# The first layer of the last experts as block products over pairs of blocks, with the token loop outermost

## The reference

```
N, D, E, F = 3072, 384, 4, 1024
p = domain_probs / (domain_probs.sum(-1, keepdims=True) + 1e-09)
for e in range(E):
    h = np.maximum(x @ w1[e], 0.0)          # first layer, 384 -> 1024
    out += p[:, e:e + 1] * (h @ w2[e])      # second layer, 1024 -> 384
```

## Time and profile before

| | |
|---|---|
| median of 3 runs | 1463.51 us (1460.65 to 1465.16) |
| the profiled execution's own time | 1463.24 us |
| its span, first to last instruction | 1461.3 us |
| mean granted clock of TensorE over the span | 0.997 |
| TensorE busy | 1430.0 us, 98% |
| VectorE, ScalarE, GpSimd busy | 609.7, 501.2, 584.0 us |

### The profile page before, as it was taken

How to read it: one execution, slowest core, us unless ns; L and a number is a source line. 1 busy time by engine, 2 the same in 40 slices (tenths; PEclk the granted TensorE clock), 3 DMA queues, 4 the chain that set the end, 5 groups by cost and what they waited for, 6 DMA issues and landing times.

```text
span 1461.3 us, 25799 instructions
## 1 busy us (share of the span) xinstructions
PE 1430.0 (98%) x10296; PEld 1319.9 (90%) x10296; DVE 609.7 (42%) x933; ACT 501.2 (34%) x975; POOL 584.0 (40%) x552
## 2 busy tenths in 40 slices
PE   4899999999999999999999999999999999999999
PEld 4889999999999999998999999999999999999998
DVE  7585556565565555113333333333333333333332
ACT  6564545454545544213222222222222222222220
POOL 6385545454454544344324323234133143232220
PEclk9999999999999999999999999999999999999999
DMA  8312222212131221110000010010010000100011
GB/s 309 116 53 104 85 72 76 81 54 102 53 102 54 85 72 33 44 44 0 1 32 13 0 44 0 0 44 0 0 43 0 23 20 0 43 0 0 22 43 65
DMA packets 31109, 70.65 MB, mean 48 GB/s; under 512 B 5168, under 2 KB 14128, under 8 KB 31024
## 3 DMA queue, kind: packets, MB, share of 16 engines
q1 hardware_dynamic: 31024, 69.43, 13.9%
HBM read 64.70 MB, written 4.72 MB: 48 GB/s over the span
## 4 chain that ended last, share of the span: by engine, by line
PE 94%; DVE 2%; ACT 2%; issue 1%; DMA 1%; SPq 0%; DVEq 0%; ACTq 0%
PE PS L671 28%; PE PS L661 27%; PE PS L617 21%; PE PS L627 10%; PE PS L565 4%; PE PS L588 2%; PE PS L584 1%; PE PS L568 1%; DMA raw<-in_w_gate 1%; ACT QX L771 1%; PE PS L573 1%; DVE KQ L883 0%; PE PS L596 0%; PE PS L601 0%; ACT AT L748 0%
## 5 line engine op out<-in xcount | busy, mean ns | idle before, releaser
L1147 POOL TENSOR_TENSOR XS_0l<-x2T,XS_0h 128x1536 fp32r<-128x1536 f32 x24 | 84.5, 3521 | 263.5 <-ACT XS_0h L816 263.5
L1037 DVE SCALAR_TENSOR_TENSOR acc<-PS,prob,acc 128x384 f32<-128x384 f32 x192 | 118.7, 618 | 162.0 <-PE PS L671 162.0
L1147 POOL TENSOR_TENSOR XS_1l<-x2T,XS_1h 128x1536 fp32r<-128x1536 f32 x23 | 80.8, 3515 | 252.5 <-ACT XS_1h L816 252.5
L771 ACT ACTIVATE QX<-KQ 48x256 f32<-48x256 f32 x288 | 120.7, 419 | 130.2 <-DVE KQ L883 107.4
L857 ACT ACTIVATE H_1h<-PS 128x512 fp32r<-128x512 f32 x96 | 57.4, 598 | 311.7 <-PE PS L661 311.7
L857 ACT ACTIVATE H_0h<-PS 128x512 fp32r<-128x512 f32 x96 | 57.3, 599 | 299.5 <-PE PS L661 299.3
L1045 DVE SCALAR_TENSOR_TENSOR H_1l<-PS,H_1h 128x512 fp32r<-128x512 f32 x96 | 66.4, 692 | 196.9 <-ACT H_1h L857 196.9
L1045 DVE SCALAR_TENSOR_TENSOR H_0l<-PS,H_0h 128x512 fp32r<-128x512 f32 x96 | 66.1, 692 | 188.7 <-ACT H_0h L857 188.7
L883 DVE TENSOR_TENSOR KQ<-KQ,TOT 112x512 f32<-112x512 f32 (+1 forms) x126 | 110.7, 902 | 46.0 <-PE PS L565 27.9
L976 DVE TENSOR_TENSOR hid<-PS,hid 128x384 f32<-128x384 f32 x96 | 53.5, 557 | 149.2 <-PE PS L617 133.8
L565 PE MATMUL PS<-QX,KQ 112*64 112x64 f32 x1920 | 82.1, 237 | 23.9 <-ACT QX L771 23.1
(11 more groups left out here) (157 smaller groups left out, 4105.0 us busy)
## 6 DMA issues: line engine op xcount, KB each, us to landing
row<-in_rows SPq DMA_DIRECT2D x24, 768.0 KB, 4.4
KQ<-in_qk SPq DMA_DIRECT2D x24, 448.0 KB, 4.1
V<-in_v SPq DMA_DIRECT2D x24, 384.0 KB, 4.8
rawA<-in_w SPq DMA_DIRECT2D x8, 768.0 KB, 4.6
rawB<-in_w SPq DMA_DIRECT2D x8, 768.0 KB, 6.3
A<-in_alpha SPq DMA_DIRECT2D x24, 224.0 KB, 2.7
out_y<-acc SPq DMA_DIRECT2D x5, 768.0 KB, 3.5
raw<-in_w_gate SPq DMA_DIRECT2D x3, 768.0 KB, 12.2
```

What stands on the lines that cost most here:

```text
L771: done = nc.scalar.activation(QX[p][rows, :, g, :].rearrange("d a (n t) -> d a n t", t=2 << level), right, ACT.Copy)
L1037: dve.scalar_tensor_tensor(out=acc[:, n, :], in0=PS[:, result_banks[u], 0:DM], scalar=weight, in1=acc[:, n, :], op0=ALU.mult, op1=ALU.add) ...
L1147: nc.gpsimd.tensor_tensor(XS[c % 2][1][:], x2T[:, :, at:at + T2], XS[c % 2][0][:].bitcast(F32), ALU.subtract).then_inc(xsl_ready, 1)
```

## The change

The unit of work becomes 1024 tokens (two halves of 512) by 256 hidden values (two blocks of 128) of one expert. The groups of 1024 tokens (`q`, three) are the outermost loop; inside are the four experts and their four units each, 48 units in all, so all weights are loaded three times.

Over two of the three blocks of `x` the first layer of a unit is the product of a 2 x 2 matrix of weight blocks and a 2 x 2 matrix of token blocks. It is computed by a scheme with seven block products instead of eight, from sums and differences of blocks: `T1_` to `T4` of `x`, `S1` to `S4` of the weights. The third block (`X31`, `X32`, `W13`, `W23`) is multiplied in the usual way and summed into the same banks. `PRODUCTS` lists the pairs of each of eight groups. The four results are sums of these groups: VectorE adds banks up in a buffer `mixed` in SBUF (`combine`), after ScalarE has copied the first product there. ScalarE rectifies a finished part twice, once into the high part `H2..h` and once in place; GpSimd subtracts (`low_h`). GpSimd also forms the sums of weights and tokens (`w_mix`, `x_mix`) and all low parts, ScalarE all high parts.

TensorE alternates one group of `first` with one block of `second` of the unit before, now eight blocks of six matmuls each; VectorE adds each block to `acc`, which now holds 1024 tokens, twice. The pieces of the next 1024 tokens (nine blocks, four of them sums) are prepared in the first units of a group after the schedule `LATER` (for each unit: blocks to split, sums to form). Those of the first group and the first weights are prepared beside the last dense tile. Stores of a finished group of tokens go out during the next one.

The diff, cut to its core (buffers, semaphores and loop ends are left out):

```diff
-FH = 512
-FCH = FH // P
+FP = 2
+UNITS = F2 // (FP * P)
 T2 = 512
-SUB = T2 // P
-TILES2 = N // T2
-PASSES = E * (F2 // FH)
+PAIR_T = 2 * T2
+SUB = PAIR_T // P
+GROUPS2 = N // PAIR_T
+ALL_UNITS = GROUPS2 * E * UNITS
...
+X11, X21, X31, T3, X22, X32, T1_, T2_, T4 = range(9)
+W11, S3, W12, W22, W13, W23, S1, S2, S4 = range(9)
+X_ORDER = (X11, X21, X31, T1_, X22, X32, T3, T2_, T4)
+T_ORDER = (T1_, T3, T2_, T4)
+PRODUCTS = (
+    ((W11, X11),),
+    ((S2, T2_),),
+    ((S3, T3),),
+    ((S1, T1_),),
+    ((W12, X21), (W13, X31)),
+    ((W22, T4), (W23, X31)),
+    ((S4, X22), (W13, X32)),
+    ((W23, X32),),
+)
+P1, P6, P7, P5, R11, R21, R12, R22 = range(8)
+COMBINED = 8
+PARTS = ((0, 0), (1, 0), (0, 1), (1, 1))
+SUMS = {P6: ((1, 0),), P7: ((2, 1),), P5: ((1, 1), (3, 2)), R11: ((0, 0),), R21: ((2, 2),), R12: ((1, 1),), R22: ((3, 3),)}
+SELF = {P7: 1, P5: 2, R12: 3, R22: 4}
...
+LATER = (((X11, X21), (T1_,)), ((X31, T1_), ()), ((X22,), (T3,)), ((X32, T3), (T2_,)), ((T2_,), ()), ((), (T4,)), ((T4,), ()), ((), ()))
...
-            def first(e, c, j, f):
-
-                wait_count(pe, rl_ready, nth(e, c, j, FCH, f + 1 - FCH))
-                for n in range(KD):
+            def first(q, e, u, g):
+
+                if g < R11:
+                    wait_count(pe, combined, nth(q, e, u, COMBINED, R11 + g + 1 - COMBINED))
+                elif g == R11:
+                    pe.wait_ge(p1_kept, nth(q, e, u, 1, 1))
+                else:
+                    pe.wait_ge(combined, nth(q, e, u, COMBINED, {R21: 1, R12: 2, R22: 4}[g]))
+                terms = [(w, x, c) for w, x in PRODUCTS[g] for c in SPLITS]
+                for at, (w, x, (cw, cx)) in enumerate(terms):
+                    mm = pe.matmul(PS[:, hidden_banks[g % 4], :], W1[u % 2][cw][:, w, :], XB[q % 2][cx][:, x, :],
+                                   start=at == 0, stop=at == len(terms) - 1)
+                mm.then_inc(first_done, 1)
...
+            def second(q, e, u, at):
+
+                wait_count(pe, acc_ready, nth(q, e, u, SUB, at + 1 - 4))
...
-                        mm = pe.matmul(PS[:, hidden_banks[f], :], W1[c // TILES2][w][:, n, f * P:(f + 1) * P],
-                                       XS[c % 2][x][:, n, :],
-                                       start=(n == 0 and (w, x) == SPLITS[0]), stop=(n == KD - 1 and (w, x) == SPLITS[-1]))
-                mm.then_inc(first_done, 1)
-
-            def second(e, c, j, u):
-
-                wait_count(pe, acc_ready, nth(e, c, j, SUB, u + 1 - SUB))
-                for f in range(FCH):
-                    for w, x in SPLITS:
-                        mm = pe.matmul(PS[:, result_banks[u], 0:DM], H2[c % 2][x][:, f, u * P:(u + 1) * P],
-                                       W2[c // TILES2 % 2][w][:, f, :],
-                                       start=(f == 0 and (w, x) == SPLITS[0]), stop=(f == FCH - 1 and (w, x) == SPLITS[-1]))
+                        mm = pe.matmul(PS[:, result_banks[at % 4], 0:DM], H2[u % 2][x][:, f, at * P:(at + 1) * P], W2[u % 2][w][:, f, :],
+                                       start=(f == 0 and (w, x) == SPLITS[0]), stop=(f == FP - 1 and (w, x) == SPLITS[-1]))
                 mm.then_inc(second_done, 1)
 
...
-                for f in pieces:
-                    first(e, c, j, f)
+            def unit(q, e, u, groups=range(len(PRODUCTS)), alone=False):
+
+                if 0 in groups:
+                    pe.wait_ge(w1_ready, nth(q, e, u, 1, 1))
+                    if u == 0 and (not isinstance(e, int) or e == 0):
+                        pe.wait_ge(xb_ready, 9 * (q + 1))
+                for g in groups:
+                    first(q, e, u, g)
                     if alone:
                         continue
-                    if f == 0:
-                        if (c - 1) % TILES2 == 0:
-                            pe.wait_ge(w2_ready, e * 2 + ((c - 1) // TILES2 + 1))
-                        pe.wait_ge(rl_ready, nth(e, c, j, FCH, 0))
-                    second(e, c - 1, j, f)
...
-            tile(B - 1, 1, attend=False, follow=False, ahead=lambda: tile2(0, 0, alone=True, pieces=range(2)))
+                    if g == 0:
+                        pe.wait_ge(w2_ready, nth(q, e, u, 1, 0))
+                        pe.wait_ge(rl_ready, nth(q, e, u, len(PARTS), 2 - len(PARTS)))
+                    if g == SUB // 2:
+                        pe.wait_ge(rl_ready, nth(q, e, u, len(PARTS), 0))
+                    second(q, e, u - 1, g)
...
+            tile(B - 1, 1, attend=False, follow=False, ahead=lambda: unit(0, 0, 0, groups=(P1, P6), alone=True))
...
-            expert(0, alone=True)
-            with pe.Fori(1, E) as e:
-                expert(e)
-            pe.wait_ge(rl_ready, PASSES * TILES2 * FCH)
-            for u in range(SUB):
-                second(E - 1, 2 * TILES2 - 1, 0, u)
+            unit(0, 0, 0, groups=range(P7, R22 + 1), alone=True)
+            pe.wait_ge(x2_ready, TILES1)
+            for u in range(1, UNITS):
+                unit(0, 0, u)
+            for q in range(GROUPS2):
+                with pe.Fori(int(q == 0), E) as e:
+                    for u in range(UNITS):
+                        unit(q, e, u)
+            pe.wait_ge(w2_ready, ALL_UNITS)
...
+            def high_w1(q, e, u):
+
+                if not (isinstance(e, int) and (q, e, u) == (0, 0, 1)):
+                    wait_count(act, first_done, nth(q, e, u, len(PRODUCTS), -len(PRODUCTS)))
+                act.wait_ge(s_ready, nth(q, e, u, 4, 4))
+                nc.scalar.activation(W1[u % 2][0][:, 0:6], rawA[u % 2][:], ACT.Copy)
+                nc.scalar.activation(W1[u % 2][0][:, 6:9], w_sum[:], ACT.Copy).then_inc(w1_high, 1)
+
+            def high_w2(q, e, u):
+
+                wait_count(act, second_done, nth(q, e, u, SUB, -SUB))
+                act.wait_ge(rawB_in[u % 2], nth(q, e, u, 1, 0) * 8 + (16 if u % 2 == 0 else 8))
+                nc.scalar.activation(W2[u % 2][0][:], rawB[u % 2][:], ACT.Copy).then_inc(w2_high, 1)
...
+            def unit(q, e, u, blocks=(), last=False):
+
+                wait_count(act, rl_ready, nth(q, e, u, len(PARTS), 1 - len(PARTS)))
+                act.wait_ge(first_done, nth(q, e, u, len(PRODUCTS), P1 + 1))
+                nc.scalar.activation(mixed[:, 0, :], PS[:, hidden_banks[0], :], ACT.Copy).then_inc(p1_kept, 1)
+                if not last:
+                    high_w1(q, e, u + 1)
+                high_w2(q, e, u)
+                for block in blocks:
+                    high_x(q + 1, block)
+                for at, (m, n) in enumerate(PARTS):
+                    act.wait_ge(combined, nth(q, e, u, COMBINED, R11 + at + 1))
+                    nc.scalar.activation(H2[u % 2][0][:, m, n * T2:(n + 1) * T2], mixed[:, part_of(m, n), :], ACT.Relu)
+                    nc.scalar.activation(mixed[:, part_of(m, n), :], mixed[:, part_of(m, n), :], ACT.Relu).then_inc(rh_ready, 1)
...
-            def add_result(e, c, u, e_of_c):
-
...
-                dve.scalar_tensor_tensor(out=acc[:, n, :], in0=PS[:, result_banks[u], 0:DM], scalar=weight,
-                                         in1=acc[:, n, :], op0=ALU.mult, op1=ALU.add).then_inc(acc_ready, 1)
-
...
+            def combine(q, e, u, g):
+
+                if g == P1:
+                    return
+                done = nth(q, e, u, COMBINED, 0)
+                bank = PS[:, hidden_banks[g % 4], :]
+                if g == P6:
+                    dve.wait_ge(p1_kept, nth(q, e, u, 1, 1))
+                    wait_count(dve, rl_ready, nth(q, e, u, len(PARTS), -1))
+                if g == P5:
+                    wait_count(dve, rl_ready, nth(q, e, u, len(PARTS), 0))
+                if g in SELF:
+                    dve.wait_ge(combined, done + SELF[g])
+                dve.wait_ge(first_done, nth(q, e, u, len(PRODUCTS), g + 1))
+                for to, x in SUMS[g]:
+                    dve.tensor_tensor(mixed[:, to, :], bank, mixed[:, x, :], ALU.add).then_inc(combined, 1)
...
+            def add_result(q, e, u, at, fresh=False):
+
+                dve.wait_ge(second_done, nth(q, e, u, SUB, at + 1))
...
+                else:
+                    dve.scalar_tensor_tensor(out=to, in0=result, scalar=weight, in1=to, op0=ALU.mult, op1=ALU.add).then_inc(acc_ready, 1)
...
+            def unit(q, e, u):
+                for g in range(len(PRODUCTS)):
+                    combine(q, e, u, g)
...
+                        add_result(q, e, u - 1, g, fresh)
...
-            def low_x(e, c):
-
-                pool.wait_ge(const_in, 16)
-                pool.wait_ge(xsh_ready, nth(e, c, 0, 1, 1))
...
-                nc.gpsimd.tensor_tensor(XS[c % 2][1][:], x2T[:, :, at:at + T2], XS[c % 2][0][:].bitcast(F32),
-                                        ALU.subtract).then_inc(xsl_ready, 1)
...
+            def x_low(q, block):
+
+                pool.wait_ge(xb_high, 9 * q + X_ORDER.index(block) + 1)
+                high, low = (t[:, block, :] for t in XB[q % 2])
```

(77 more changed lines are left out.)

257 lines of the change are left out of this document (127 added, 130 removed).

## The result

| | before | changed |
|---|---|---|
| median | 1463.28 us (1460.65 to 1465.16, 4 runs) | **1438.3 us** (1436.23 to 1439.41, 4 runs) |
| ratio | | 0.9829, 95% interval 0.981 to 0.9848 |
| profiled execution: time, span | 1463.24, 1461.3 | 1438.04, 1436.2 |

The forecast was 1439 (1438.8 for the profiled execution), its range 1428 to 1453. In a second set, on another chip, the changed kernel took 1437.67 us, ratio 0.983 (0.9817 to 0.9844).

What follows compares the result with a forecast made beforehand. TensorE, busy for 98% of the span, was taken to bound the kernel. From 1463.24 us, -33.4 + 0.8 + 0.3 + 6.5 + 1.4 = -24.4 gave 1438.8, as a median 1439 us, range 1428 to 1453.

Steps and rivals of the forecast that it cites:

- The matmuls: Expert stage on TensorE: 144 first-layer matmuls go at 0.232 us each, -33.4 us, leaving a unit of 16.07 us.
- The start: First unit of the stage: GpSimd has no head start, so TensorE waits from 661.6 for low part h1, +6.5 us.
- the end is the same chain: End of the kernel: last block, addition of 0.62 us and DMA of 192 KB as before, at no cost.
- P1: Start of the stage: TensorE waits for R11's bank until ScalarE has kept the first product, +0.3 us.
- The clock: After the idle at the start TensorE resumes at the 1.2 GHz level: +1.4 us, at most 2.8.
- Units with three token pieces: Three such units inside the stage: pieces ahead on GpSimd's queue make h1 late by up to 0.3 us, +0.8 in all.
- A: Rival: matmul groups on TensorE cost something at each change, +0.24 us a unit, +12, so 1451 us; chance 0.12.
- B: Rival: GpSimd is 10 to 15% slower than its profile rows, delaying h1 and the start: 1448 us; chance 0.10.
- C: Rival: GpSimd's queue becomes the bound from a stretch of 1.29; 128-wide L1076 showed 1.71; about 1700 us; chance 0.11.
- D: Rival: small waits of half a microsecond in each unit give the saving back: within 0.3% of 1463; chance 0.03.
- So the loss isn't repeated: After the start's wait, GpSimd ends h1 of unit 1 at 683.6 and TensorE wants it from 684: no second wait.
- The work beside the last dense tile: First token splits and weights are hidden beside the last dense tile at no cost; +4 us should this cover fail.

Runs made afterwards that it cites:

- Experiment 1: Changed kernel with P1's three matmuls issued twice in every unit, so 36 first-layer matmuls as before the change: 1470.41 us, ratio 1.0055 to the kernel before.
- experiment 9: Changed kernel with weights and P1 of unit 0 made before the dense layer ends, and token pieces spread over units 2 to 10: 1429.02 us, ratio 0.9776.
- Experiment 6: Changed kernel with three more unused 768-column GpSimd subtractions in each unit: 1581.18 us, ratio 1.0817 to the kernel before.
- experiment 7: Changed kernel with two unused 512-wide VectorE additions, both operands in SBUF, in each unit: 1444.15 us, ratio 0.9873 to the kernel before.
- experiments 2 to 4: Changed kernel, cumulatively: first unit's low parts of H before token pieces, 1437.19 us; first unit's weights split earlier, 1434.86; P1 kept before x2T's copy, 1435.03.
- experiments 8 and 9: Changed kernel with token pieces at most two a unit, units 2 to 10: 1433.8 us; also unit 0's weights and P1 made earlier: 1429.02 us.

## Why the prediction was right

**The matmuls.** Forecast: -33.4, a unit of 16.07. From the stage's 780.5 us take the two waits (6.2 and 0.4) and the low clock (1.7, below): 772.2 for 48 units, 16.09 each. 805.6 - 772.2 = 33.4. Experiment 1 puts the saving back and finds the tile of before to 0.01 us (16.77 in all three token groups, so the three matmuls are worth 0.70 us in two of them and 0.67 in the other). This is the whole of the gain.

**The start.** Forecast: the second low part of H at 668.1, TensorE idle from 661.6 for 6.5 us. Measured: 667.27, and a hole of 6.2. The steps stand in the chain with nearly constant distance: low parts of the first weights done 659.34 (660.1 forecast), second weights 661.15 (661.9), pieces 664.82 (665.6). All are 0.8 early, 0.64 of it because the stage began at 650.60 instead of 651.24, an offset of the execution (in experiment 9 the stage began at 651.36); what follows the last matmul took 0.6 longer (3.5 for 2.9 us of the span), so that the two cancel. The second is no offset: every profile of a changed kernel has it, and "the end is the same chain" put it at nothing. Its cause wasn't looked for.

**P1.** Forecast +0.3, measured 0.4.

**The clock.** Forecast +1.4. Experiment 9, whose granted clock is 1.00 there, has this first block behind its 0.6 us hole:

```profile
661.96 1.30 PE PS L748 x6
```

So 0.25 of the excess belongs to resuming and not to the clock. In the changed kernel the first four pieces are 2.26, 1.15, 1.04 and 0.70: 1.2 and 0.45 over their later lengths, 1.7 in all, 1.4 without the 0.25. That the earlier trace rows gave the same figure for another hole (1.61 us of idle) is partly luck: the drop doesn't follow the length of the hole alone (last section).

**Units with three token pieces.** Forecast +0.8 (three units, each late by up to 0.3; 3 x 0.3 would be 0.9), mis-sized: no wait in the list. But it was close. In the first of the three, the low parts of H ran like this:

```profile
714.43 3.79 POOL L1305 TENSOR_TENSOR H_1l<-mixed,H_1h 128x512 fp32r<-128x512 f32 x3
```

The second of these three ended at 716.97, and TensorE started on it at 717.12; in the other two units the lead was 0.28 and 0.21 us, where plain units have 2.5. From the end of the last unit's low part to this one the layout has 14.5 us and the trace 14.1. Half of the difference is the four weight sums, laid out at 2.0 us and measured at 1.8, as one starts about 0.05 us before the last one ends (above, 673.62 + 1.86 is 675.48, and the next starts at 675.43); the rest is a few hundredths at each later step.

**Sum.** -33.4 + 6.2 + 0.4 + 1.7 = -25.1; the span went from 1461.3 to 1436.2, which is -25.1. Forecast: -24.4. The terms differ by -0.8 (three pieces), -0.3 (the start), +0.1 (P1) and +0.3 (the clock), so part of the agreement is errors that offset one another.

**The rivals.** A (groups cost something at each change, +12): not so, as the unit is 16.07 to 16.10 and experiment 1's is 16.77. B (GpSimd 10 to 15% slower): its rows kept their lengths to 1%. C (GpSimd the bound, 1700): a stretch of 1.29 was its point and 1.00 was measured. Experiment 6 shows that the mechanism exists, experiment 7 what kind of operation would have brought it about. The doubt about the 128-wide operation (785 ns in another place) is settled for this form: 463. D: two waits, not 48.

**The step that was right for another reason than the one given.** "So the loss isn't repeated", the prediction says of the hole, with TensorE asking at 684 for what is ready at 683.6. That was right (ready at 682.6, wanted at 685.1), but I carried it on into the expectations of experiments 2 to 4 as if GpSimd would be in time in unit 1 in any case. At the start it is in time only after a hole. Later it carries the same load: unit 1 of the second token group has the same two pieces, behind a unit with three, and its low part is 1.0 us early. Only moving the pieces of units 0 and 1 away (experiments 8 and 9) gives the gain of a shorter hole in full; which of the five matter was not tried.

**The work beside the last dense tile.** Costed at nothing, 4 us had its cover failed. The stage began no later than before, so it held.

## What to carry to other kernels

Where one engine fills the chain and the rest is hidden, work taken off it is worth its full time, and the risk is in round trips: lay out one period of every queue with its hand-overs, then the first period once more, without a lead. A hole at a start is also the lead of a queue behind it; before closing it, ask which queued work the hole let pass, and move that too. And when work moves to VectorE beside a busy GpSimd, look where its operands are: with one in PSUM the two engines didn't touch each other, with both in SBUF each slowed the other.
